# A retention, MLP and gated-MLP chain in float32 on one Trainium2 core: warm-up products, the first hidden unit and the place of T4

## What is computed

```python
# 1. retention: q, k, v of shape (2, 8, 768, 64), per head gamma = 1 - 2**(-5-h)
for t in range(S):
    state = gamma * state + outer(k[t], v[t])
    y[t] = (1 / sqrt(64)) * q[t] @ state
x = y.transpose(0, 2, 1, 3).reshape(1536, 512)
# 2. first MLP, d_ff = 2048
h = x @ w_in                        # 512 -> 2048
x = (h * sigmoid(1.702 * h)) @ w_out
# 3. gated MLP with RMS norm, d_ff = 1536
xn = x / sqrt(mean(x * x) + 1e-6) * rms_g
g = xn @ w_gate
out = (g * sigmoid(g) * (xn @ w_val)) @ w_out
```

## Time and profile before

| | us |
|---|---|
| median of three runs | 584.25 (584.05 to 584.41) |
| the profiled execution, its own time | 583.44 |
| its span, first to last instruction | 581.6 |
| TensorE busy | 573.3 |
| VectorE / ScalarE / GpSimd busy | 359.2 / 298.1 / 172.1 |

### The profile page before, as it was taken

One profiled execution on the slowest core, in us unless ns is written; L12 is line 12 of the kernel. 1 busy time (PEld: TensorE's weight loads), 2 busy tenths in 40 slices (PEclk: granted clock), 3 DMA queues, 4 the chain that ended last, 5 costly groups with the idle time before them and its releaser, 6 DMA issues.

```text
span 581.6 us, 9400 instructions
## 1 busy us (share of the span) xinstructions
PE 573.3 (99%) x3640; PEld 551.8 (95%) x3640; DVE 359.2 (62%) x486; ACT 298.1 (51%) x501; POOL 172.1 (30%) x222
## 2 busy tenths in 40 slices
PE   7999999999999999999999999999999999999997
PEld 7988999999999999999999999998889999998886
DVE  5797555676425667775346768678755666666432
ACT  1244766645336766645237655574444555564321
POOL 2386444000222452000314464410051545420000
PEclk9999999999999999999999999999999999999999
DMA  8981222322112222312202222233213322224202
GB/s 319 392 292 37 74 72 73 108 73 73 38 36 73 72 74 70 111 39 72 73 0 74 73 74 72 74 84 99 73 36 125 93 73 73 73 74 112 69 1 108
DMA packets 24220, 52.84 MB, mean 91 GB/s; under 512 B 1776, under 2 KB 1904, under 8 KB 24176
## 3 DMA queue, kind: packets, MB, share of 16 engines
q1 hardware_dynamic: 23600, 50.41, 28.2%
q10 hardware_dynamic: 576, 1.84, 0.8%
HBM read 49.09 MB, written 3.15 MB: 90 GB/s over the span
## 4 chain that ended last, share of the span: by engine, by line
PE 97%; DVE 1%; DMA 1%; issue 0%; ACT 0%
PE bank L539 20%; PE twin L539 20%; PE twin L480 11%; PE twin L483 11%; PE twin L482 11%; PE bank L483 6%; PE bank L480 6%; PE bank L482 6%; PE twin L392 2%; PE bank L438 2%; PE bank L425 1%; DMA arena<-attn_in 1%; PE bank L409 1%; DVE x_lo L787 0%; PE bank L580 0%
## 5 line engine op out<-in xcount | busy, mean ns | idle before, releaser
L778 DVE TENSOR_TENSOR w_lo<-raw,w_hi 128x512 fp32r<-128x512 f32 (+2 forms) x148 | 149.3, 1024 | 49.7 <-ACT w_hi L612 49.5
L1059 POOL TENSOR_TENSOR raw<-raw 128x256 f32<-128x256 f32 x40 | 32.1, 803 | 317.1 <-DMA raw<-w 312.5
L480 PE MATMUL twin<-x_hi,w_hi 128*128 128x384 f32 x360 | 120.5, 335 | 0.6 <-ACT arena L676 0.6
L483 PE MATMUL twin<-x_hi,w_lo 128*128 128x384 f32 x360 | 120.3, 334 | 0.0
L482 PE MATMUL twin<-x_lo,w_hi 128*128 128x384 f32 x360 | 120.2, 334 | 0.0
L612 ACT ACTIVATE w_hi<-raw 128x512 fp32r<-128x512 f32 (+2 forms) x148 | 109.0, 763 | 18.0 <-PE bank L539 7.6
L813 DVE TENSOR_TENSOR g_lo<-arena,g_hi 128x768 fp32r<-128x768 f32 x56 | 54.3, 970 | 74.8 <-ACT g_hi L642 74.8
L642 ACT ACTIVATE g_hi<-arena 128x768 fp32r<-128x768 f32 x56 | 47.5, 848 | 103.6 <-PE bank L539 103.6
L480 PEld LDWEIGHTS twin<-x_hi,w_hi 128*128 128x128 f32 x360 | 67.6, 188 | 0.9 <-ACT arena L676 0.9
L482 PEld LDWEIGHTS twin<-x_lo,w_hi 128*128 128x128 f32 x360 | 67.6, 188 | 0.0
L483 PEld LDWEIGHTS twin<-x_hi,w_lo 128*128 128x128 f32 x360 | 67.6, 188 | 0.0
(11 more groups left out here) (105 smaller groups left out, 995.9 us busy)
## 6 DMA issues: line engine op xcount, KB each, us to landing
raw<-w SPq DMA_DIRECT2D x68, 512.0 KB, 3.7
arena<-attn_in SPq DMA_DIRECT2D x22, 512.0 KB, 7.9
out<-x SPq DMA_DIRECT2D x1, 1536.0 KB, 8.6
out<-x SPq DMA_DIRECT2D x6, 256.0 KB, 2.0
arena<-attn_in ACTq DMA_DIRECT2D x2, 512.0 KB, 10.1
arena<-tables ACTq DMA_DIRECT2D x1, 512.0 KB, 6.1
arena<-tables ACTq DMA_DIRECT2D x1, 256.0 KB, 9.8
ident<-ident_in SPq DMA_DIRECT2D x1, 64.0 KB, 12.8
```

Source lines behind the costliest of these rows:

```text
L480: pe.matmul(dst, w_hi[q][:, w], x_hi[:, x], start=start and kk == 0, stop=False, skip_group_check=True)
L483: mm = pe.matmul(dst, w_lo[q][:, w], x_hi[:, x], start=False, stop=kk == 1, skip_group_check=True)
L778: dve.tensor_tensor(w_lo[q % 3][:, dst], src, w_hi[q % 3][:, dst].bitcast(F32), ALU.subtract)\
L1059: pool.tensor_tensor(s1, a21, a22, ALU.add).then_inc(w_sums, 1)
```

## The change

`WARM_UP` goes from 8 to 11 and `FILL` with its loop is removed. In unit 0 TensorE makes M6 before M3, so the order becomes M1, M5, M2, M6, M3, M7. In the list `LOWER` of the first phase T2 comes before T3, as VectorE now lowers them in that order. T4's sum moves on VectorE from the start of unit 0 to right behind T2's sum, and the third piece of the weights behind the two lowerings. On ScalarE the conversion of T4 moves behind the first piece of unit 1's weights and `copy_u2`. `lower_x(0, T4)` on VectorE keeps its place, ahead of `lower_next`.

```diff
--- before.py
+++ after.py
@@ -22,8 +22,7 @@
 FF1, FF2 = 2048, 1536
 NF1, NF2 = FF1 // P, FF2 // P
 EPS = 1e-6
-WARM_UP = 8
-FILL = 3
+WARM_UP = 11
 
 
 T_MASK = HEADS + PAIRS
@@ -52,7 +51,7 @@
 UPPER = {True: (B11, B21, B22, T1, T3, T2, T4), False: (B11, B21, T1, T2, B22, T3, T4)}
 
 
-LOWER = {True: (B11, B21, T1, B22, T3, T2, T4), False: (B11, B21, T1, T2, B22, T3, T4)}
+LOWER = {True: (B11, B21, T1, B22, T2, T3, T4), False: (B11, B21, T1, T2, B22, T3, T4)}
 
 
 SET = ((0, 1, 2), (3, 4, 5))
@@ -446,10 +445,6 @@
                 pe.matmul(gate[1][:, 0:P], ones[:, :], ones[:, :], start=True, stop=True)
             for a in range(0, STEPS, 2):
                 scores(a)
-                if a == 0:
-
-                    for _ in range(FILL):
-                        pe.matmul(gate[1][:, 0:P], ones[:, :], ones[:, :], start=True, stop=True)
                 scores(a + 1)
                 if a == 0:
                     new_products(0)
@@ -514,9 +509,9 @@
                     pe.wait_ge(m1_copied, n + 1)
                     product(2, n, 0, 0, 2, B21, False)
                     pe.wait_ge(w_lo_done, lo_at[r] + 2)
+                    product(6, n, 2, 1, 2, T2, False)
                     pe.wait_ge(m5_copied, n + 1)
                     product(3, n, 1, 1, 3, B22, False)
-                    product(6, n, 2, 1, 2, T2, False)
                 pe.wait_ge(u2_copied, n + 1)
                 pe.wait_ge(w_lo_done, lo_at[r] + 3)
                 product(7, n, 2, 1, 0, T3, False)
@@ -730,10 +725,10 @@
                     copy_m5(n)
                     if j > 0 and not is_val(n - 1):
                         activate(n - 1, 3)
+                    split_next(r, 0)
+                    copy_u2(n)
                     if n == 0:
                         split_x(0, T4)
-                    split_next(r, 0)
-                    copy_u2(n)
                     if not is_val(n):
                         activate(n, 0)
                     split_next(r, 1)
@@ -948,9 +943,10 @@
                     new_state(a + 2)
                 if a == 10:
                     sum_x(0, T2)
+                    sum_x(0, T4)
+                    lower_x(0, T2)
+                    lower_x(0, T3)
                     lower_w(0, 2)
-                    lower_x(0, T3)
-                    lower_x(0, T2)
 
 
             for p, (layer, _) in enumerate(PHASES):
@@ -961,7 +957,6 @@
                     if n > 0:
                         lower_w(r, 1)
                     else:
-                        sum_x(0, T4)
                         lower_x(0, T4)
                     if j > 0 and is_val(n - 1):
                         gate_tile(n - 1, 2)
```

## The result

| | before | changed |
|---|---|---|
| median of 20 runs each, us | 584.32 (583.52 to 585.61) | 585.21 (584.38 to 587.94) |
| ratio, 95% interval | | 1.002 (1.0013 to 1.0027) |
| profiled execution / its span | 583.44 / 581.6 | 584.57 / 582.8 |

The changed kernel is slower by 0.2%: 0.89 us by the medians, 1.17 by the ratio, 1.13 by the two profiled executions. Beside the kernel before on another occasion (9 runs) it took 585.81 against 584.24, a ratio of 1.0039 (1.0022 to 1.0056).

What follows compares the result with a forecast made beforehand. It took TensorE, busy 573.3 of 581.6 us, as the bound, with transfers pacing the attention part. 0 - 0.85 + 2.39 = +1.54 on the median 584.25 gave 585.8, rounded down to 585.7; range 584.2 to 586.5.

Steps and rivals of the forecast that it cites:

- The front: Longer warm-up, no fill, in the attention part: value 0, because loads pace it; bounds -1.6 to +0.3 us.
- M3 between M6 and M7: First hidden unit of the dense part: copy_u2 runs inside M3, so M7 starts without a wait; -0.85 us.
- T4's words: Dense entrance: T4's late conversion and lowering delay the second unit's first weight residual, and TensorE waits; +2.39 us.
- three sizes: Loss at the second unit: +1.36 with VectorE alone, +1.90 with VectorE ahead of POOL, +2.39 with POOL first.
- rival (a): At the dense entrance VectorE's pair goes first or unhindered: 585.3 or 584.8 us; chance 0.25.
- Rival (b): TensorE paces the attention part, so the front brings up to 2.6 us: 583.2; chance 0.05 whole, 0.07 in part.
- (d): The change does only what it says and T4's order is harmless: -0.85, 583.4 us; chance 0.08.
- Rival (c): TensorE's clock falls to 1.2 GHz in the new 2.2 us gap at 57 us: 588.6 us; chance 0.05.

Runs made afterwards that it cites:

- experiment 2: Eleven warm-up products and no fill, on the kernel before, the rest as it was: 584.38 us against 584.11, ratio 1.0000.
- experiment 3: Changed kernel with the old front back (eight warm-up, three fill products): 586.46 us, ratio 1.0041; on a second occasion 585.71, ratio 1.0032.
- experiment 7: Second unit's weights loaded later, on the kernel before with M6 ahead of M3 (ratio 0.9988) and on the changed kernel with ScalarE's old order (0.9985).
- Experiment 1: Kernel before with only the swap, M6 ahead of M3 in the first hidden unit: 583.45 us against 584.11, ratio 0.9988.
- longer gap: Changed kernel with TensorE at the second unit waiting for the second piece of the weights' residual too: 588.52 us, ratio 1.0077.
- filled gap: Changed kernel with six 128x128 products of ones before TensorE's wait at the second unit: 585.65 us, ratio 1.0021.
- experiments 4: Changed kernel with ScalarE's order put back, T4's conversion ahead of the next weights and copy_u2: 583.38 us against 584.11, ratio 0.9990.
- experiment 5: Changed kernel with VectorE's lowering of T4 moved behind the second unit's first residual and c12: 583.54 us against 584.45, ratio 0.9986.
- experiment 8: Changed kernel with TensorE's stop at the second unit made longer (588.52 us, ratio 1.0077) or filled with six products (585.65, 1.0021).

## Why the prediction was right

**The front: 0.** Right in size, and for the reason given up to 24 us: 1.28 us idle at 23.80 where there were 0.34, and experiments 2 and 3 put it at nothing. For the later wait, at 44 us, I gave the transfers alone as the reason, and experiment 7 shows VectorE behind them. The first scores did run at the 2.4 GHz level (1.16 us). The granted clock was 0.50 from 8.6 to 11.9 us in this execution, so the second scores took 2.08 as before; in the changed kernel's other profile they took 1.16, and nothing came of that either.

**M3 between M6 and M7: -0.85.** The copy ran at 55.10 (forecast 55.06) and M7 had no wait. Experiment 1 measured the swap alone at ratio 0.9988, 0.7 us; 0.85 lies inside its interval (0.2 to 1.2 us).

**T4's words: +2.39, of the three sizes 1.36, 1.90 and 2.39.** The mechanism held; the term was mis-sized, since I took the wrong one of the three for this execution. T4's conversion began at 55.49 (forecast 55.45), VectorE at 56.36 (56.32), but POOL, waiting for the third unit's weights, began at 56.92, not at 56.2. The step that failed is the time at which VectorE is done with the attention part. I took T2's sum at 48.12, as in the one profile before, and it began 0.7 us later, so the load was issued at 53.12, not 52.45. The row before and the two after (the last holds two loads, the first of them at 53.12):

```profile
48.12 0.95 DVE L804 TENSOR_TENSOR x<-t,x 128x768 f32<-128x768 f32 x1
...
48.81 0.94 DVE L799 TENSOR_TENSOR x<-t,x 128x768 f32<-128x768 f32 x1
...
53.12 9.11 SPq L338 DMA_DIRECT2D raw<-w  x2
```

VectorE went first, as in rival (a), and the residual was ready at 58.73 (58.68 in that case): 1.91 lost. The other two sizes were seen too: with POOL held 1.38 lost (1.36), and with POOL first, in experiment 3's profile, 61.08 - 58.91 + 0.11 = 2.28 (2.39). All agree with a model in which the two engines take turns whole instructions long.

Which of the two sizes comes isn't fixed by the edit. In both profiles of the changed kernel, in experiment 3's second one and in that of the longer gap, T2's sum begins 1.6 us ahead of the entry and VectorE goes first. In experiment 3's first profile and in the filled gap's it begins 2.3 us ahead, as before, and POOL goes first (in the filled gap at 56.91 against 57.04, with 2.37 lost). Experiment 1, with VectorE's old order, has the 1.6 too. So the 0.7 us is a difference between executions, and one profile of before could not tell which it would be.

**Sum and chances.** Forecast 585.7, measured 585.21 and, on the second occasion, 585.81; slower and in range. On the first the outcome is rival (a)'s 585.3. That the second lies on the forecast is luck: its profile shows rival (a)'s wait too, with a later entry. Rival (b), TensorE pacing the attention part, is out by experiment 2, and (d), T4 harmless, by experiments 4 and 5. Rival (c), the clock, I gave 0.05 with a fall in every execution; in both profiles of the changed kernel it is absent, and experiment 8 shows it after a stop twice as long at the same place.

## What to carry to other kernels

When an instruction is moved to cure a wait, follow what stands behind it in its engine's queue, and then the queue of the engine that takes its result. Here the swap alone gave the 0.7 to 0.85 us, and T4's conversion, moved behind the copy, cost 1.9. When an operand becomes ready later on one engine, its consumer's place in the next engine's queue must move too (experiment 5), or it blocks what stands behind it. Time won ahead of a full transfer queue was paid back here as idleness at the next load (1.28 us for 0.34). And where a forecast hangs on which of two engines starts first by a tenth of a microsecond, look at the same place in several executions before choosing.

## What the runs showed of the hardware

VectorE's tensor_tensor with both inputs in SBUF and GpSimd's take turns, a whole instruction each. The same 128x768 residual took 0.95 us with GpSimd silent and 1.49 beside it. T4's lowering and the residual together took 1.83 us with GpSimd held, 2.37 with VectorE first (changed kernel) and 2.74 with GpSimd first by 0.2 us (experiment 3). The Trainium skill, page "SBUF — State Buffer", section "SBUF: two separate sides", describes this pair of ports as an exclusive lock for whoever starts first; these rows agree.

TensorE's granted clock was at 0.50 when the engine went on at 60.7 after 3.56 us of idleness, and in no profile after the stops of 1.1 to 2.0 us at 57 to 61. At the start of the kernel the same stop did and did not go with a fall: with the new front TensorE stood 1.3 to 1.5 us before the second scores in all nine profiles, and the clock was at 0.50 near 9 to 11 us in four of them. Experiment 1, with the old front, has it at 0.50 from 7.9 us, in the middle of products that ran without a stop (its last stop, 1.97 us, had ended at 6.65). So which idleness brings the fall isn't shown.
